# An attention, expert and gated-MLP kernel: first pair split head by head, inverse sums ahead of the key split, queries scaled by heads, token placing dealt over four steps

## What is computed

```python
scores = scale * np.matmul(q, k.transpose(0, 1, 3, 2))
thresh = np.max(scores, axis=-1, keepdims=True) - tau
scores = np.where(scores >= thresh, scores, -1000000000.0)
scores = scores - np.max(scores, axis=-1, keepdims=True)
attn = np.exp(scores)
attn = attn / (np.sum(attn, axis=-1, keepdims=True) + 1e-09)
return np.matmul(attn, v)
...
for s in range(S):
    fresh_e = int(np.argmax(logits[b, s]))
    if s == 0 or local_gate[b, s] < 0.5:
        e = fresh_e
    else:
        e = prev_e if prev_e >= 0 else fresh_e
    ...
    out[b, s] = p[e] * (np.maximum(x[b, s] @ w1[e], 0.0) @ w2[e])
```

## Time and profile before

| what | value |
|---|---|
| median of 3 runs | 995.79 us (994.01 to 1001.41) |
| profiled execution, its own time | 996.88 us |
| its span in the trace | 994.8 us |
| PE busy | 900.2 us (90%) |
| DVE busy | 563.0 us (57%) |
| ACT busy | 414.4 us (42%) |
| POOL busy | 382.8 us (38%) |
| attention, 0 to 382 us: PE / DVE / ACT / POOL busy | 330.40 / 267.48 / 230.24 / 164.99 us |
| mean granted share of TensorE's clock | 0.972 |

### The profile page before, as it was taken

How to read it: one execution, slowest core, us unless ns; L and a number is a source line. 1 busy time by engine, 2 the same in 40 slices (tenths; PEclk the granted TensorE clock), 3 DMA queues, 4 the chain that set the end, 5 groups by cost and what they waited for, 6 DMA issues and landing times.

```text
span 994.8 us, 16236 instructions
## 1 busy us (share of the span) xinstructions
PE 900.2 (90%) x5991; PEld 760.0 (76%) x5991; DVE 563.0 (57%) x1203; ACT 414.4 (42%) x777; POOL 382.8 (38%) x347
## 2 busy tenths in 40 slices
PE   4798998899889986599999999999969999999996
PEld 3677787788768875488888887788858889788895
DVE  5677767776777765724657568760024525345252
ACT  4566666566656652133333333333323212132130
POOL 2454434634563232445565555555204004040000
PEclk9899999899999998799999999999979999999999
DMA  5322332232223013542665466630030020110101
GB/s 122 90 67 61 74 95 68 65 95 74 60 61 108 14 60 133 196 133 85 193 195 161 158 198 196 192 105 27 2 108 1 1 96 1 48 49 1 48 1 47
DMA packets 47643, 86.79 MB, mean 87 GB/s; under 512 B 8012, under 2 KB 16332, under 8 KB 47568
## 3 DMA queue, kind: packets, MB, share of 16 engines
q1 hardware_dynamic: 43568, 76.32, 26.8%
q0 software_dynamic: 4000, 9.45, 2.9%
HBM read 73.42 MB, written 15.99 MB: 90 GB/s over the span
## 4 chain that ended last, share of the span: by engine, by line
PE 50%; DVE 6%; DMA 4%; issue 1%; ACT 1%; POOL 0%; DVEq 0%; POOLq 0%
PE ps_h L1313 4%; PE ps_y L1332 4%; PE ps_h L1315 4%; PE ps_y L1334 4%; PE ps_h L1314 4%; PE ps_y L1333 4%; PE ps_a L1595 4%; PE ps_a L1597 4%; PE ps_a L1596 4%; PE ps_v L1595 3%; DMA w_raw<-in_w 3%; PE ps_v L1597 2%; PE ps_v L1596 2%; DVE w_low L1253 2%; PE ps_r L1595 2%; PE ps_r L1596 2%
## 5 line engine op out<-in xcount | busy, mean ns | idle before, releaser
L490 ACT COPY probs_t<-ps_ring 128x512 f32<-128x512 f32 (+1 forms) x192 | 105.9, 560 | 117.3 <-PE ps_ring L579 103.7
L780 DVE SCALAR_TENSOR_TENSOR probs<-ps_s,floor,expd 128x576 f32<-128x576 f32 x144 | 117.0, 813 | 62.9 <-ACT expd L447 62.7
L533 PE MATMUL ps_s<-k_high,q_split 128*128 128x288 f32 x336 | 108.6, 341 | 29.3 <-DVE probs L780 15.6
L1245 DVE CAST w_high<-w_raw 128x1024 fp32r<-128x1024 f32 (+1 forms) x63 | 65.0, 1048 | 98.6 <-PE ps_h L1315 50.4
L447 ACT ACTIVATE expd<-ps_s,max_tau 128x576 f32<-128x576 f32 x144 | 107.8, 749 | 12.5 <-DVE max_tau L766 12.4
L766 DVE TENSOR_REDUCE max_tau<-ps_s 128x1 f32<-128x576 f32 x144 | 106.7, 741 | 0.8 <-PE ps_s L534 0.8
L533 PEld LDWEIGHTS ps_s<-k_high,q_split 128*128 128x128 f32 x336 | 65.8, 196 | 50.5 <-DVE probs L780 29.2
L610 PE MATMUL ps_ring<-probs_t,v_pair 128*64 128x144 f32 x1280 | 92.6, 292 | 10.3 <-ACT probs_t L490 10.3
L534 PE MATMUL ps_s<-k_low,q_split 128*128 128x288 f32 x336 | 94.0, 302 | 0.0
L610 PEld LDWEIGHTS ps_ring<-probs_t,v_pair 128*64 128x64 f32 x1280 | 76.0, 137 | 21.8 <-ACT probs_t L490 13.3
L1472 POOL TENSOR_TENSOR rstd<-var_eps,exponent 128x1 f32<-128x1 f32 (+1 forms) x20 | 17.2, 860 | 180.2 <-DVE var_eps L1534 180.2
(11 more groups left out here) (235 smaller groups left out, 2046.9 us busy)
## 6 DMA issues: line engine op xcount, KB each, us to landing
w_raw<-in_w SPq DMA_DIRECT2D x64, 512.0 KB, 4.1
q_in<-in_q SPq DMA_DIRECT2D x32, 288.0 KB, 4.3
k_in<-in_k SPq DMA_DIRECT2D x32, 288.0 KB, 5.6
v_pair<-in_v SPq DMA_DIRECT2D x16, 256.0 KB, 2.7
x_rows_dram<-scratch SPq DMA_DIRECT2D x4, 1024.0 KB, 4.5
out<-scratch SPq DMA_DIRECT2D x4, 1024.0 KB, 4.3
scratch<-in_dense SPq DMA_DIRECT2D x8, 384.0 KB, 5.8
scratch<-y_rows_dram SPq DMA_DIRECT2D x3, 1024.0 KB, 5.5
```

The source lines that it names most:

```text
L533: nc.tensor.matmul(out, lhs, k_high[par][:, h, cols], start=first, stop=False)
L780: nc.vector.scalar_tensor_tensor(out=row_of(pair, w).rearrange("p (a c) -> p a c", a=2), in0=scores(n), scalar=floor[:, n % 4:n % 4 + 1], ...
```

## The change

What it does, part by part:

1. Start. Pair 0's q and k are loaded head by head, in the order q0, k0, tau, q1, k1, and scaled, rounded and split head by head, with semaphores of their own. DVE sets all its constants ahead of this. PE begins with 16 products of a tile of ones (`keep_warm`), into a bank that the first item overwrites. The waits for the constants and the padded values move from PE's first instruction to step `MAIN_AT`.
2. POOL runs `spread(pair - 1)` ahead of `split_k(pair + 1)`. SP loads k of a pair as soon as k of the one before is split, and q when q is.
3. `scale_q` runs for one head at w2 and for the other at w3, in place of both at w1.
4. The placing: `place_tokens` stays at step 38 with its first two instructions; `within_tiles` (the other three) goes to step 42 (39 for batch 2), `add_run` one step behind, `chosen_probs` two steps behind. The item "ids" goes from step 46 to 48.

```diff
-ARGMAX_AT, SPREAD_AT, CHOOSE_AT, CHOSEN_AT, PLACE_AT, IDS_AT = 26, 28, 32, 37, 38, 46
+ARGMAX_AT, SPREAD_AT, CHOOSE_AT, CHOSEN_AT, PLACE_AT, IDS_AT = 26, 28, 32, 37, 38, 48
+WITHIN_AT = (42, 42, 39)
+SCALE_AT = (2, 3)
+START_FILLS = 16
...
-        load_qk(0)
-        sp.dma_start(tau[:], io["tau"].to_broadcast([P, 1])).then_inc(tau_loaded, 16)
+        for h in range(2):
+            for half in range(2):
+                sp.dma_start(q_in[DH * half:DH * half + DH, h, :], q_dram[0, h]).then_inc(q_loaded if h else q_first, 16)
+            for half in range(2):
+                sp.dma_start(k_in[DH * half:DH * half + DH, h, :], k_dram[0, h]).then_inc(k_loaded if h else k_first, 16)
+            if h == 0:
+                sp.dma_start(tau[:], io["tau"].to_broadcast([P, 1])).then_inc(tau_loaded, 16)
...
         sp.wait_ge(k_ready, 1)
+        load_k(1)
         sp.wait_ge(q_ready, 1)
-        load_qk(1)
+        load_q(1)
...
                 sp.wait_ge(k_ready, pair + 2)
+                load_k(pair + 2)
                 sp.wait_ge(q_ready, pair + 2)
-                load_qk(pair + 2)
+                load_q(pair + 2)
...
         for pair in range(ALL_PAIRS):
+            if pair > 0:
+                spread(pair - 1)
             if pair + 1 < ALL_PAIRS:
                 split_k(pair + 1)
-            if pair > 0:
-                spread(pair - 1)
...
-            nc.scalar.mul(q_in[:], q_in[:], float(DH) ** -0.5).then_inc(q_scaled, 1)
+            nc.scalar.mul(q_in[:, h, :], q_in[:, h, :], float(DH) ** -0.5).then_inc(q_scaled, 1)
...
-            if w == 1 and pair + 1 < ALL_PAIRS:
-                scale_q(pair + 1)
+            for h in range(2):
+                if w == SCALE_AT[h] and pair + 1 < ALL_PAIRS:
+                    scale_q(pair + 1, h)
...
+        def keep_warm(count, bank):
+
+            for _ in range(count):
+                nc.tensor.matmul(bank.rearrange("p (a c) -> p a c", a=4), ones[:], ones[:].unsqueeze(1).to_broadcast([P, 4, P]),
+                                 start=True, stop=True)
...
         if steps.start == 0:
-            pe.wait_ge(const_loaded, 32)
-            pe.wait_ge(v_padded, 4)
+            pe.wait_ge(ones_set, 1)
+            keep_warm(START_FILLS, ps_r[:, 0, :])
             score(0)
...
-        dve.wait_ge(k_loaded, 32)
-        nc.vector.tensor_copy(k_high[0][:], k_in[:]).then_inc(k_cast, 1)
-        dve.wait_ge(k_cast, 1)
-        nc.vector.tensor_tensor(k_low[0][:], k_in[:], k_high[0][:].bitcast(F32), ALU.subtract).then_inc(k_ready, 1)
-        dve.wait_ge(q_cast, 1)
-        dve.wait_ge(set_up, 2)
-        low = q_halves(0, slice(DH, P))
-        nc.vector.tensor_tensor(low, q_in[DH:P, :, :], low.bitcast(F32), ALU.subtract).then_inc(q_ready, 1)
...
+        for h in range(2):
+            dve.wait_ge(k_loaded if h else k_first, 32)
+            nc.vector.tensor_copy(k_high[0][:, h, :], k_in[:, h, :]).then_inc(first_high, 1)
+            dve.wait_ge(first_high, h + 1)
+            nc.vector.tensor_tensor(k_low[0][:, h, :], k_in[:, h, :], k_high[0][:, h, :].bitcast(F32), ALU.subtract).then_inc(k_ready if h else first_low, 1)
+            dve.wait_ge(first_cast, h + 1)
+            if h == 0:
+                dve.wait_ge(set_up, 2)
+            low = q_head(h, slice(DH, P))
+            nc.vector.tensor_tensor(low, q_in[DH:P, h, :], low.bitcast(F32), ALU.subtract).then_inc(q_ready if h else first_low, 1)
...
                     if n == after_batch(b, PLACE_AT):
                         place_tokens(b)
+                    if n == after_batch(b, WITHIN_AT[b]):
+                        within_tiles(b)
+                    if n == after_batch(b, WITHIN_AT[b] + 1):
                         add_run(b)
+                    if n == after_batch(b, WITHIN_AT[b] + 2):
                         chosen_probs(b)
```

More of the change, by code:

```diff
@@ L277, in attention, with q_head @@
     block = big.enter_context(nc.Block())
-    POOL_CONSTS, DVE_CONSTS = 10, 9
+    POOL_CONSTS, DVE_CONSTS = 10, 8
     def q_halves(par, part):
         return q_split[par][part].rearrange("p (h s) -> p h s", h=2)[:, :, 0:S]
+    def q_head(h, part):
+        return q_split[0][part, (S + TAIL) * h:(S + TAIL) * h + S]
     def scores(n):
@@ L299, in _, with load_q, load_k @@
     def _(sp):
-        def load_qk(pair):
+        def load_q(pair):
             for half in range(2):
                 sp.dma_start(q_in[DH * half:DH * half + DH, :, :], q_dram[pair].rearrange("h d s -> d h s")).then_inc(q_loaded, 16)
+        def load_k(pair):
             for half in range(2):
@@ L372, in split_k @@
             nc.gpsimd.tensor_copy(k_high[par][:], k_in[:]).then_inc(k_cast, 1)
-            pool.wait_ge(k_cast, pair + 1)
+            pool.wait_ge(k_cast, pair)
             nc.gpsimd.tensor_tensor(k_low[par][:, 0, :], k_in[:, 0, :], k_high[par][:, 0, :].bitcast(F32), ALU.subtract)
@@ L379, in split_q @@
             par = pair % 2
-            pool.wait_ge(q_scaled, pair + 1)
+            pool.wait_ge(q_scaled, 2 * pair)
             nc.gpsimd.tensor_copy(q_halves(par, slice(0, P)), q_in[:]).then_inc(q_cast, 1)
-            pool.wait_ge(q_cast, pair + 1)
+            pool.wait_ge(q_cast, pair)
             low = q_halves(par, slice(DH, P))
@@ L438, in scalar_steps, with scale_q @@
     def scalar_steps(act, steps, row_banks=None):
-        def scale_q(pair):
+        def scale_q(pair, h):
             act.wait_ge(q_loaded, 32 * pair + 32)
-            nc.scalar.mul(q_in[:], q_in[:], float(DH) ** -0.5).then_inc(q_scaled, 1)
+            nc.scalar.mul(q_in[:, h, :], q_in[:, h, :], float(DH) ** -0.5).then_inc(q_scaled, 1)
         def exp_scores(n):
@@ L505, in scalar_steps @@
         if steps.start == 0:
-            scale_q(0)
-            act.wait_ge(q_scaled, 1)
-            nc.scalar.copy(q_halves(0, slice(0, P)), q_in[:]).then_inc(q_cast, 1)
+            for h in range(2):
+                act.wait_ge(q_loaded if h else q_first, 32)
+                nc.scalar.mul(q_in[:, h, :], q_in[:, h, :], float(DH) ** -0.5).then_inc(first_scaled, 1)
+                act.wait_ge(first_scaled, h + 1)
+                nc.scalar.copy(q_head(h, slice(0, P)), q_in[:, h, :]).then_inc(first_cast, 1)
         for n in steps:
@@ L538, in score @@
             par = pair % 2
-            if w == 0:
+            if n == 0:
+                pe.wait_ge(first_low, 2)
+            if w == 0 and n > 0 or n == 1:
                 pe.wait_ge(k_ready, pair + 1)
@@ L685, in tensor_steps @@
                 score(n + 1)
+            if n == MAIN_AT:
+                pe.wait_ge(const_loaded, 32)
+                pe.wait_ge(v_padded, 4)
             for k, item in enumerate(STEPS[n]):
@@ L725, in vector_begins @@
         nc.vector.memset(route["slot_col"][:, SLOTS:SLOTS + 2], 0).then_inc(consts, 1)
+        for h in range(2):
+            dve.wait_ge(k_loaded if h else k_first, 32)
[7 more added lines that the diff above has]
+            nc.vector.tensor_tensor(low, q_in[DH:P, h, :], low.bitcast(F32), ALU.subtract).then_inc(q_ready if h else first_low, 1)
+        dve.wait_ge(tau_loaded, 16)
+        nc.vector.tensor_copy(max_tau[:, :, 1], tau[:].to_broadcast([P, 4])).then_inc(set_up, 1)
         dve.wait_ge(set_up, 5)
```

8 lines of the change are left out of this document (5 added, 3 removed).

## The result

The changed kernel takes 984.01 us (median of 4 runs, 983.58 to 986.12), the kernel before beside it on the same chip 997.62 us (4 runs): ratio 0.9871, 95% interval 0.9847 to 0.9895. By the ratio it is 1.3% faster, by the two medians 13.6 us. I had forecast 979, in a range of 970 to 988. Its profiled execution, the slowest of the four, took 986.12 us, with a span of 984.3; before, 996.88 and the earlier trace rows. In those two traces the first mask of the last pair (unit 135) starts at 327.48 us in place of 344.66: 17.2 us gained in the attention, against 17.8 forecast. The end comes only 10.5 us earlier, so 6.7 us are lost behind it.

The account below looks back on a forecast made before the run. PE was taken as the engine to keep fed, 1.7 us idle in a 20.05 us pair. Terms 3.0 + 0.7 + 5.0 + 2.3 + 4.4 + 3.2 + 1.2 - 2.0 = 17.8 us off 996.88 gave 979, range 970 to 988.

Parts of the forecast that it names:

- the halves: Query scaling by heads: PE waits less at w2, part returns at w4; 0.15 us a pair, 2.3 us over 15 pairs.
- Start: Loading and splitting by heads brings the first row maximum at 10.7 in place of 13.77: 3.0 us gained.
- Rival five: Start gives nothing, as loads land later and the clock falls in the pause: 983 us, inside the range, no chance stated.
- The 0.7 for the warmed clock: Pair 0: warming products may bring PE to full clock early; up to 1.5 us or nothing, taken as 0.7.
- Pair 1: Spread ahead of the key split removes PE's wait for the inverse sums and the lower clock behind it: 5.0 us.
- the rival at 968: Half scalings cost nothing downstream: a steady pair takes 19.2 us and not 19.9, the time is 968; chance 0.13.
- Placing: Pairs 8 and 12: moving the small DVE instructions to where POOL is idle gains 4.4 and 3.2 us.
- Argmax and scan: POOL's moved splits: argmax in pairs 6 and 10 gains 1.2 us, scan in pairs 7 and 11 loses 2.0.
- POOL late: Query split ends past the score of w0, PE waits in each of 15 pairs: 1009 us; chance 0.03.
- The rest keeps its length: Everything after the attention, the first 382 us, passes on its gain or loss unchanged; no term was given to it.

Follow-up runs that it names:

- e12: Changed kernel with the old start (first pair whole, constants behind, no warming products), k of pair 1 still loaded ahead of q: 979.90 us, ratio 0.9799.
- e6: Changed kernel with q of pair 1 loaded ahead of k of pair 1: 979.32 us, ratio 0.9805.
- e8: Changed kernel without the 16 warming products at the start: 982.35 us, ratio 0.9859.
- e2: Changed kernel with the spread of the inverse sums behind the key split again: 983.83 us, ratio 0.9864.
- e5: Changed kernel with q and k of a pair loaded together behind both splits, q first, spread still ahead: 984.71 us, one run.
- e9: Changed kernel with q and k loaded together behind both splits and the spread behind the key split: 986.08 us, one run.
- e4: Changed kernel with the queries scaled in one instruction of both heads at w1 again: 988.13 us, ratio 0.9910.
- e7: Changed kernel with both half scalings of the queries at w2: 980.63 us, ratio 0.9815.
- e11: Changed kernel with q of pair 1 first, no warming products, both half scalings at w2 except in pairs 7 and 11: 977.64 us, ratio 0.9784.
- e3: Changed kernel with the placing in one piece at w2 again and the item ids at step 46: 988.23 us, ratio 0.9916.
- e1: The changed kernel run once more, nothing altered: 983.14 us, ratio 0.9878.

## Why the prediction was right, and where it was not

The forecast of faster held, and the time lies in the range. The gain forecast was 17.8 us; 17.2 of it came in the attention, and by the medians 13.6 in the whole. By stretches, each with the 0.15 us a pair of the halves in the forecast, the earlier start of mask 135 came out so:

| stretch | forecast | measured |
|---|---|---|
| start and pair 0 | 3.0 + 0.7 + 0.15 = 3.85 | 2.93 - 1.99 = 0.94 |
| pair 1 (stall) | 5.15 | 4.44 |
| pairs 2 to 5 | 0.6 | 1.33 |
| pairs 6, 10 (argmax) | 1.5 | 2.43 |
| pairs 7, 11 (scan) | -1.7 | -0.35 |
| pair 8, pair 12 (placing) | 4.55, 3.35 | 4.67, 3.58 |
| pairs 9, 13 | 0.3 | -0.37 |
| pair 14 | 0.15 | 0.49 |
| sum | 17.75 | 17.2 |

- **Start: wrong.** The 3.0 us came, at 10.84 against 10.7, and went again. The step that failed is the sentence "SP issues k's load after the k split, ahead of q's, some 15 us before it is wanted. This is hidden." It holds for a steady pair. In pair 0 nothing is loaded ahead: the next queries are wanted as soon as they land, I had taken nothing off that path, and with k in front they land later still. Rival five ("the start gives nothing") was nearly the case, and the wait for these loads, which I had not named, is one reason: e12 puts the start's worth at 0.3 us, e6 shows 1.3 us more for the order of two loads. The 0.7 for the warmed clock was nothing (e8): the clock did come up, and fell again at 12.0 us, soon after the pause, much as the rival had it; how much of pair 0's growth is clock stays open.
- **Pair 1: right in size, wrong in cause.** 4.4 us against 5.0. I put it all on the spread's place; e2, e5 and e9 show two parts each of which removes the stall alone, the other being the early load of k, which I had costed at nothing.
- **Halves: right in mechanism, too small.** Gain at w2, loss at w4, both as described; 0.36 us by e4 and not 0.15. The mis-sized term is what comes back at w4: from mask to mask w1 became 0.81 us shorter (forecast 0.8), w3 only 0.49 longer, where I had counted 0.6 and a little more. e7 shows why: without the half in front PE waits 0.20 for that bank, with it 0.67. So the loss was avoidable as well. e7's steady pair of 19.24 is the 19.2 of the rival at 968 (nothing comes back), but its 11 us were not there to be had: e11, with that pair and no long scan, has mask 135 4.5 us ahead of the changed kernel, 1.6 of it from queries first and no fills by their single runs.
- **Placing: right.** Pairs 8 and 12 at 21.55 and 21.51 (forecast 21.85, less 0.15). e3 gives 5.6 us back when this part alone is undone, of 8.25 gained in the two pairs; the rest is shared with the other parts, since in e3 the piece meets the key split and not the query split. I had read one waiting instruction in the piece, and there were two. Ahead of `within_tile` stood

```profile
185.80 1.00 DVE L877 TENSOR_SCALAR place_up<-place 128x5 f32<-128x5 f32 x1
```

which ends with POOL's cast of 185.63 (1.15 us), and takes 0.16 in the changed kernel. The clock fell at 192.3, while PE still stood, not behind the wait.

- **Argmax and scan: direction right, the scan mis-sized.** The scan met the query split as feared, by 0.65 us of it only, and took 0.5 and not 1.1 us longer. e2 shows that with the loads apart it is the spread's place that spares pairs 6 and 10 0.75 us each (forecast 0.6); the other 0.5 of their 1.2 are the halves, by e4 (22.34). But e9 spares them as much with the spread behind and the loads joined, so the order by itself is not the cause: it is whether the key split is still running when the argmax comes, and that shifts with all that moves the two. Pairs 9 and 13 lost 0.37 us where I had 0.3 of gain, and no run takes that apart. By the page SBUF — State Buffer of the Trainium skill ("Who interferes with whom") an instruction of DVE with two SBUF inputs and one of GpSimd that reads SBUF contend; the scan (1.85 and 2.16 against 1.33) agrees. e3's `tile_at` (1.37 us) and the `place_up` above (1.00), with one tensor input in SBUF, waited too, which that sentence of the page does not cover.
- **POOL late:** did not come; in pair 3 the query split ends at 80.86, and PE first scores with it at 85.19: 4.3 us of slack, as forecast (4).
- **"The rest keeps its length": wrong.** From mask 135 to the end the profiled executions took 650.1 us before and 656.8 after. By the medians the gain missed the forecast by 4.2 us, and 3.6 of them lie behind mask 135: this is the term I had put at nothing. Of the 6.7 us of the two traces, 3.3 lie in the tail. PE in the tail before, then after:

```profile
371.73 3.23 PE L624 MATMUL ps_ring<-w_route,scratch 128*128 128x9 f32 x29 [0.15 <-ACT probs_t L490]
...
374.87 3.87 PE L610 MATMUL ps_ring<-probs_t,v_pair 128*64 128x144 f32 x59
```

```profile
354.56 3.92 PE L649 MATMUL ps_ring<-w_route,scratch 128*128 128x9 f32 x29 [0.15 <-ACT probs_t L510]
...
358.44 6.40 PE L635 MATMUL ps_ring<-probs_t,v_pair 128*64 128x144 f32 x59
```

The same instructions, as far behind the mask of unit 143 (7.1 us), but at half clock from 356.8 to 363.6 us. Two further falls (404.6 and 961.0 us) lie in the rest of the loss, and did not come again in e1. Over the runs the whole gain by the medians was smaller than that of mask 135 by 2.1 to 4.1 us in the changed kernel and in e1 to e8, where there are several runs, equal to it in e11 (21.7 and 21.7), and larger in e12 (20.8 and 16.9), each on its chip. In the profiled execution, then, 3.3 us are clock that PE lost in the tail. That all of the 2 to 4 us of the medians are clock is not shown: e3 loses 2.9 with no fall in its tail, and mask 135 of the kernel before is known from a single trace. What decides whether the clock falls there stays open too.

## What to carry to other kernels

When a start is made shorter, look for the next transfer that waits for the same buffers: a gain in front of it dies there (2.93 us gained, 1.99 given back, and the order of two loads decides over 1.3 us). When one instruction is moved off a wait, put it where its engine is idle and nobody is queued behind it, and check each stretch that has other work in it (e7 won 0.49 us in a plain pair and lost 1.3 in two others). Undo parts in pairs as well as one at a time: of two parts that each remove the same stall, either looks worthless when it alone is undone (pair 1: 18.66 and 18.64 us with one undone, 23.82 with both).

## What the runs showed of the hardware

- Small DVE instructions held up by POOL end with POOL's instruction: `place_up` 1.00 us and `within_tile` 2.62 before, `tile_at` 1.37 and `run` 1.15 in e3, each to within 0.1 us of the end of a cast or a subtraction of POOL. These take 0.16 to 0.18 with POOL idle. Others beside the same work took their usual time (`hot_sum` 0.21 in e3), so not every overlap costs.
- In the tail the clock fell in 12 of 14 traces, while PE multiplied on 9 columns or up to 0.5 us after, with hardly a pause (at most 0.49 us behind the mask of unit 143 in the changed kernel). In e6 a first fall, at 350.8 us, came 4 us ahead of these products. There was no fall in the kernel before and in e3, where the same instructions stand at the same distance from the mask of unit 143 (7.09 us, as in 11 of the 12 others). A fall lasted 3.4 or 6.8 us in all and cost 1.6 or 3.3 us.
- The stretch from mask 135 to the end, the same instructions throughout, took from 649.2 to 658.3 us in the 14 traces, and was at half clock for 37.9 to 54.1 us of it. The two go together only loosely (38.1 us and 652.2 in e1, 43.8 and 649.2 in e3), so the clock is not the whole of that spread.
